# Queries, keys and decay of the first attention phase loaded as rows 0 to 63 and rows 64 to 111

## What is computed

```python
for t in range(S):
    state = alpha[:, :, t, :, None] * state + np.einsum('bhd,bhe->bhde', k[:, :, t], v[:, :, t])
    y[:, :, t] = np.einsum('bhd,bhde->bhe', q[:, :, t], state)
```

## Time and profile before

| | |
|---|---|
| median of 3 runs | 735.87 us (734.6 to 736.44) |
| profiled execution, its own time | 734.97 us |
| span from its first to its last instruction | 733.2 us |
| TensorE busy | 700.5 us, 96% |
| VectorE, ScalarE, GpSimd busy | 54%, 46%, 29% |
| DMA, mean | 67 GB/s |

### The profile page before, as it was taken

How to read it: one execution, slowest core, us unless ns; L and a number is a source line. 1 busy time by engine, 2 the same in 40 slices (tenths; PEclk the granted TensorE clock), 3 DMA queues, 4 the chain that set the end, 5 groups by cost and what they waited for, 6 DMA issues and landing times.

```text
span 733.2 us, 25693 instructions
## 1 busy us (share of the span) xinstructions
PE 700.5 (96%) x11336; PEld 662.1 (90%) x11336; DVE 395.6 (54%) x668; ACT 338.8 (46%) x573; POOL 210.8 (29%) x141
## 2 busy tenths in 40 slices
PE   2688899999999999999999999999999999999998
PEld 2688789899998999999999899998998998999998
DVE  6888674554764554655553314224943851870671
ACT  5787546445546446446435331334532432532422
POOL 6504490320350220161120231452360051033022
PEclk9979999999999999999999999999999999999999
DMA  9414401311401131301000251002100101101001
GB/s 360 163 47 151 176 4 46 120 40 43 154 3 46 45 112 46 132 25 46 23 16 2 92 155 69 33 1 97 64 34 33 65 12 54 64 1 64 0 0 65
DMA packets 16525, 49.49 MB, mean 67 GB/s; under 512 B 1616, under 2 KB 9552, under 8 KB 15920
## 3 DMA queue, kind: packets, MB, share of 16 engines
q1 hardware_dynamic: 16432, 48.09, 18.6%
HBM read 38.65 MB, written 9.44 MB: 66 GB/s over the span
## 4 chain that ended last, share of the span: by engine, by line
PE 90%; DVE 3%; issue 1%; ACT 1%; DVEq 0%
PE HB L886 25%; PE ZB L963 7%; PE ZB L965 7%; PE ZB L964 7%; PE SB L886 6%; PE SB L1000 5%; PE SB L763 4%; PE ZB L886 4%; PE SB L868 2%; PE SB L1004 2%; PE ZB L1013 2%; PE ZB L1000 2%; PE SB L877 2%; PE SB L823 2%; PE SB L1013 2%; PE HB L1000 1%
## 5 line engine op out<-in xcount | busy, mean ns | idle before, releaser
L1523 DVE SCALAR_TENSOR_TENSOR hid_lo<-HB,hid_hi 128x384 fp32r<-128x384 f32 x96 | 53.3, 556 | 139.4 <-ACT hid_hi L1199 138.4
L1199 ACT ACTIVATE hid_hi<-HB 128x384 fp32r<-128x384 f32 x96 | 47.2, 492 | 156.3 <-PE HB L886 156.1
L886 PE MATMUL HB<-uh,w1h 128*128 128x384 f32 x288 | 103.1, 358 | 2.6 <-DVE ul L1519 1.5
L963 PE MATMUL ZB<-hid_hi,w2h 128*128 128x384 f32 x288 | 98.6, 342 | 0.0
L886 PE MATMUL HB<-ul,w1h 128*128 128x384 f32 x288 | 96.7, 336 | 0.0
L965 PE MATMUL ZB<-hid_lo,w2h 128*128 128x384 f32 x288 | 96.6, 336 | 0.0
L886 PE MATMUL HB<-uh,w1l 128*128 128x384 f32 x288 | 96.5, 335 | 0.0
L964 PE MATMUL ZB<-hid_hi,w2l 128*128 128x384 f32 x288 | 96.3, 334 | 0.0
L1054 ACT COPY Qd<-Q 48x768 f32<-48x768 f32 x84 | 73.0, 869 | 13.6 <-PE SB L763 5.2
L713 POOL TENSOR_TENSOR gl<-gf,gh 128x384 fp32r<-128x384 f32 x32 | 33.5, 1047 | 144.1 <-ACT gh L1239 143.8
L656 POOL TENSOR_TENSOR Q<-Q,bk 112x768 f32<-112x768 f32 x13 | 24.8, 1905 | 174.2 <-ACT Qd L1054 174.2
(11 more groups left out here) (260 smaller groups left out, 1500.8 us busy)
## 6 DMA issues: line engine op xcount, KB each, us to landing
Q<-in_q SPq DMA_DIRECT2D x8, 768.0 KB, 5.8
AL<-in_al SPq DMA_DIRECT2D x7, 768.0 KB, 4.4
K<-in_k SPq DMA_DIRECT2D x7, 768.0 KB, 4.3
Vt<-in_v SPq DMA_DIRECT2D x8, 576.0 KB, 3.7
mid<-x2s SPq DMA_DIRECT2D x8, 576.0 KB, 4.1
x<-mid SPq DMA_DIRECT2D x4, 1152.0 KB, 5.2
out<-o_sb SPq DMA_DIRECT2D x24, 192.0 KB, 1.8
x2s<-in_w SPq DMA_DIRECT2D x9, 384.0 KB, 4.4
```

The costliest lines, as they stand in the source:

```text
L886: last = nc.tensor.matmul(dst, weights(x, w), moving(y, m), start=(n == 0 and x == y == 0), stop=(n == total - 1 and y == 1))
L963: nc.tensor.matmul(bank, w2h[:, i, cols], hi, start=(i == 0), stop=False)
L1199: nc.scalar.activation(hid_hi[:, i % HID, :], HB[i % 2][:, 0:TILE], ACT.Relu).then_inc(h_hi, 1)
L1523: nc.vector.scalar_tensor_tensor(hid_lo[:, i % HID, :], HB[i % 2][:, 0:TILE], 0.0, hid_hi[:, i % HID, :].bitcast(F32), ALU.max, ALU.subtra ...
```

## The change

The first loads of `Q`, `K` and `AL` of both groups (`first=True`, six tensors of 128 x 1536 fp32, 768 KB each) become two loads each: rows 0 to 63 (384 KB) and rows 64 to 111 (288 KB). Rows 112 to 127 are no longer loaded there. Later loads keep their 128 rows. A first tensor now adds 32 to its semaphore, so all waits on these three count 16 more (`rows_loaded`).

```diff
+FIRST_ROWS = [slice(0, ROW1), slice(ROW1, ROWS)]
...
+        def rows_loaded(a):
+            return 16 * (len(FIRST_ROWS) + a)
...
+            def load_rows(dst, src, loaded, parts):
+                for r in parts:
+                    sp.dma_start(dst[r, :], src[r, :]).then_inc(loaded, 16)
...
-                sp.dma_start(space(a, g).whole_k[:, :], k[a, g]).then_inc(ld_k[g], 16)
+                load_rows(space(a, g).whole_k, k[a, g], ld_k[g], FIRST_ROWS if first else [slice(0, P)])
...
-                sp.dma_start(whole_q[g][:, :], q[a, g]).then_inc(ld_q[g], 16)
+                load_rows(whole_q[g], q[a, g], ld_q[g], FIRST_ROWS if first else [slice(0, P)])
...
-                sp.dma_start(space(a, g).whole_al[:, :], al[a, g]).then_inc(ld_al[g], 16)
+                load_rows(space(a, g).whole_al, al[a, g], ld_al[g], FIRST_ROWS if first else [slice(0, P)])
...
-                pe.wait_ge(ld_k[g], 16)
+                pe.wait_ge(ld_k[g], rows_loaded(0))
...
-                dve.wait_ge(ld_al[g], 16)
+                dve.wait_ge(ld_al[g], rows_loaded(0))
```

More of the change, by code:

```diff
@@ L534, in load_decay @@
                     sp.wait_ge(al_used[pg], pa + 1)
-                sp.dma_start(space(a, g).whole_al[:, :], al[a, g]).then_inc(ld_al[g], 16)
+                load_rows(space(a, g).whole_al, al[a, g], ld_al[g], FIRST_ROWS if first else [slice(0, P)])
             def load_group(a, g):
                 load_decay(a, g, False)
-                sp.wait_ge(ld_al[g], 16 * (a + 1))
+                sp.wait_ge(ld_al[g], rows_loaded(a))
                 load_queries(a, g, False)
-                sp.wait_ge(ld_q[g], 16 * (a + 1))
+                sp.wait_ge(ld_q[g], rows_loaded(a))
                 load_values(a, g)
@@ L544, in load_group @@
                 load_keys(a, g, False)
-                sp.wait_ge(ld_k[g], 16 * (a + 1))
+                sp.wait_ge(ld_k[g], rows_loaded(a))
             def load_piece(n):
@@ L593, in _ @@
             load_decay(1, 0, False)
-            sp.wait_ge(ld_al[0], 32)
+            sp.wait_ge(ld_al[0], rows_loaded(1))
             load_keys(1, 0, False)
-            sp.wait_ge(ld_k[0], 32)
+            sp.wait_ge(ld_k[0], rows_loaded(1))
             for n in range(W1_PIECES, W1_PIECES + STAGE):
@@ L599, in _ @@
             load_queries(1, 0, False)
-            sp.wait_ge(ld_q[0], 32)
+            sp.wait_ge(ld_q[0], rows_loaded(1))
             load_values(1, 0)
@@ L606, in _ @@
                 load_queries(b + 1, 1, False)
-                sp.wait_ge(ld_q[1], 16 * (b + 2))
+                sp.wait_ge(ld_q[1], rows_loaded(b + 1))
                 load_values(b + 1, 1)
@@ L610, in _ @@
                 load_decay(b + 1, 1, False)
-                sp.wait_ge(ld_al[1], 16 * (b + 2))
+                sp.wait_ge(ld_al[1], rows_loaded(b + 1))
                 load_keys(b + 1, 1, False)
-                sp.wait_ge(ld_k[1], 16 * (b + 2))
+                sp.wait_ge(ld_k[1], rows_loaded(b + 1))
                 store_mid(b, range(0, 1))
@@ L786, in att_step @@
                     if n == 0:
-                        pe.wait_ge(ld_k[g], 16 * (a + 1))
+                        pe.wait_ge(ld_k[g], rows_loaded(a))
                     else:
@@ L1061, in att_start @@
                 pa, pg = before(a, g)
-                act.wait_ge(ld_q[g], 16 * (a + 1))
+                act.wait_ge(ld_q[g], rows_loaded(a))
                 if first:
@@ L1362, in att_start @@
             def att_start(a, g):
-                dve.wait_ge(ld_al[g], 16 * (a + 1))
+                dve.wait_ge(ld_al[g], rows_loaded(a))
                 pa, pg = before(a, g)
```

## The result

The changed kernel takes 744.66 us (median of 4 runs, 743.1 to 745.46), the kernel before 735.77 us beside it: a ratio of 1.0104, 95% interval 1.0076 to 1.0133, so 5.6 to 9.8 us slower; the medians lie 8.9 us apart. The profiled execution took 743.1 us with a span of 741.3, 8.1 us more than before in both.

The account below looks back on a forecast made before the run. TensorE, busy 96% of the span, was taken as the bound, behind a start chain of loads, then VectorE. The profiled 734.97 + 4.8 us delay = 739.8, with the execution 0.9 under the median: 740.6 us; range 734.8 to 744.2.

Parts of the forecast that it names:

- rival B: First six loads: everything at 198 GB/s, `K_side` 8.9 us late, the chain 8.65, kernel 744.5 us; chance 0.11.
- TensorE is full from 70 us on and passes the start's delay on unchanged: From 70 to 732 us TensorE is busy 654.7 of 662 us, so the start's +4.8 us reaches the end one to one.
- The rate, not the issuing, spaces the landings; the row span sets the rate: First loads: bandwidth of 415 GB/s spaces landings 1.92 us apart; six more issues cost nothing; loads under 128 rows run slower.
- The low rate read from `V_in`: Kernel before, 20.5 to 24 us: `V_in`'s 96 rows ran at 198 GB/s if the loss is put down to it alone.
- The 64-row half, 1.99 us: Each first tensor's rows 0 to 63 load at the slow rate of 198 GB/s, taking 1.99 us.
- The 48-row half, 0.85 us: Each first tensor's rows 64 to 111 take 0.85 us, near the fast end of 0.71 to 1.49; 2.84 us a tensor together.
- The first tensor, 0.45 us late: Start of the kernel: the first tensor is through at 4.9 us instead of 4.5, 0.45 us late.
- the slack of 0.25: Group 1's start: `K_side` can land 0.25 us later before VectorE's `take` of group 1 is delayed.
- The chain behind `K_side`: `K_side` lands 5.05 us late, at 19.65; VectorE's `take` of group 1 and all behind it move by 4.8 us.
- Rival A: First loads keep 415 GB/s and bytes count: kernel 735.2 us, not slower, no measurable change; chance 0.20.
- Rival C: The slow-clock stretch at 44 to 48 us moves or vanishes, giving 3 us back: 737.6 us; chance 0.09, shared with overlap.

Follow-up runs that it names:

- experiment 4: Changed kernel with the six loads of rows 64 to 111 issued on ScalarE's own queue: ratio 1.0114 to the kernel before, one execution of 2345 us left out.
- experiment 5: Changed kernel with only group 0's three first tensors split into rows 0 to 63 and 64 to 111, group 1's loaded as 128 rows: 742.18 us, ratio 1.0100.
- experiment 1: Changed kernel with each first tensor loaded as two loads of 128 rows x 768 columns, nothing left out: 736.84 us, ratio 1.0010 to the kernel before.
- experiment 2: Changed kernel with each first tensor loaded as rows 0 to 63 and 64 to 127, no rows left out: 746.77 us, ratio 1.0152 to the kernel before.
- experiment 8: Changed kernel with each first tensor loaded as rows 32 to 95, 0 to 31 and 96 to 127: 741.84 us, ratio 1.0080 to the kernel before.
- experiment 7: Kernel before with `V_in` loaded as 128 rows (384 KB for 288): 734.73 us in one run.
- experiment 3: Changed kernel with each first tensor loaded in one load of rows 0 to 111, not split: 737.56 us, ratio 1.0024 to the kernel before.

## Why the prediction was right, and where it was off

The direction was the one forecast, and in the main the mechanism too. The size is that of rival B (744.5), not of the forecast (740.6). The ratio, 1.0104, applied to the 735.87 us that the prediction started from gives 743.5 us, inside the range of 734.8 to 744.2; the median itself, 744.66, lies 0.5 us above its end. The forecast's own interval, 737.9 to 742.5, holds neither: what holds the ratio is the part added for rival B. Step by step:

**TensorE is full from 70 us on and passes the start's delay on unchanged.** Right. The `take` of group 1 is 8.1 us late and the span 8.1 us longer. In the seven experiments on the first loads the difference of the medians (in experiment 4 without the execution of 2345 us) follows the lateness of that `take` within 1.2 us; single executions stray further (experiment 5).

**The rate, not the issuing, spaces the landings; the row span sets the rate.** Right (experiments 1, 2, 8). I had costed the six issues at nothing. Experiment 1 puts six more issues, with shorter packets, at 1.1 us of start and 0.7 us of time, an interval that holds zero.

**The low rate read from `V_in`.** Right, and experiment 7 settles what I had left open, that the short packets might carry part of it.

**The 64-row half, 1.99 us.** In the changed kernel `K_side`'s 64 rows land at 7.21 + 14.4 = 21.6 us and its 48 rows at 7.72 + 15.3 = 23.0, after `AL_side` was whole at 6.6 + 13.1 = 19.7: 1.9 us for the one, 1.4 for the other. `K`'s land 2.0 and 1.3 us behind `AL`, with the 48 KB of `masks` between. The first term was sized rightly.

**The 48-row half, 0.85 us.** This is the step that failed: "after a slow load the engines no longer march together, so some write upper rows while others write the lower rows of the next tensor". The half took 1.3 to 1.4 us, near its upper end of 1.49. The windows above stay at 214 to 224 GB/s, and even two queues of opposite halves gave 190 (experiment 4), so halves side by side do not help each other as I had supposed. Together this makes 3.2 to 3.3 us a tensor for 2.84.

**The first tensor, 0.45 us late.** Also too low: `Q` is whole at 6.7 us, 1.7 late. Of the 1.2 us beyond my 0.45, the longer 48-row half accounts for 0.5. The doubled issues hardly do: in experiment 1 ScalarE starts on `Q` at 5.17 us for 5.05 before, in the changed kernel at 6.77. The rest was not taken apart.

Sum as measured: (23.0 - 6.7)/5 = 3.26 us a tensor, 1.34 more than before, and 1.7 + 5 x 1.34 = 8.4 us for `K_side`, less the slack of 0.25: 8.1.

**The chain behind `K_side`.** Right where all six or group 1's three are split. With group 0's alone, and just so with two queues, `K` and VectorE's unbroken work behind it took the place of `K_side` (experiments 5 and 4).

**Rival A** fell: the halves run at 214 to 224 GB/s, and even 112 rows in one load only at 301. **Rival B**, which I gave 0.11, was right in its number, and in its argument but for the first tensor, to which it gave 1.1 us. That argument is the Trainium skill's, SBUF — State Buffer, section "Can I just issue two DMAs to hit both halves?", that two loads to the two halves serialize; the rates of experiments 2 and 4 agree. **Rival C**, the clock: the slow stretch is absent indeed; where the earlier trace rows show 0.50, the changed kernel has

```profile
50.00:60.00 10.00, 8.43 (x182) 8.05 (x176) 9.00 (x15) 9.23 (x19) 0.00 (x0) 1.00 0.09 26
```

with ScalarE and VectorE now the full ones. It gave back 0.5 us and not 2 to 3: the first L832 product comes 8.6 us later than before (50.49 for 41.88), the first of L877 8.2 (61.19 for 53.03). I had misread its price. The L823 groups, which I took to be slow by the clock, take 2.82 and 2.58 us in the changed kernel at a granted clock of 1.00 (there L832). The transposes behind them do get shorter (the first ten 1.18 us for 2.13), but then TensorE waits 1.36 us for VectorE. Nor need the change have taken the slow stretch away: the kernel of experiment 7, whose first phase is that of before, has 1.00 from 44 to 48 us too, and its L868 products start at 52.88 for 53.03.

No version that leaves rows out beats the kernel before: a 128-row load of 768 KB with 16 empty rows (1.92 us) is quicker than each way of loading 112 rows that was tried (2.3 us in one piece, 3.3 in two).

## What to carry to other kernels

Zeros that fill a load up to 128 rows can be cheaper than leaving them out: what counts is bytes by rate, and the rate hangs on which rows a load covers. Before trimming the rows of a load that something waits for, look in the trace for a load with fewer rows and read GB/s, not the share of busy DMA engines, in the stretch in which it flows. And where several loads must land before a chain can go on, cost the delay at the last of them: the bandwidth lost on every earlier one adds up there. Then look whether an earlier landing with much unbroken work behind it, as `K` in experiments 4 and 5, has become the later chain.

## What was unexpected of the hardware

A load of 96 rows amid loads of 128 pulled the rate of all down to 274 GB/s for 1.5 us and 383 for 2 more, also that of the full loads around it. The queries' 64-row load takes 0.62 us to issue on SyncE in experiment 4, where their 128-row load takes 0.40 before. And a single gap of 1.4 us inside TensorE's dense stretch, with no releaser, came in some executions and not in others, so that one profiled execution can be off by nearly as much as experiment 3 had to tell.
